# A fused attention and expert kernel on one core: first loads put first on their queue, the embeddings' small operations moved to the end of the attention, and the last two steps' products taken by row block

## The reference, cut to what matters

```python
scores = scale * np.matmul(q, k.transpose(0, 1, 3, 2))
thresh = np.max(scores, axis=-1, keepdims=True) - tau
scores = np.where(scores >= thresh, scores, -1000000000.0)
...
en = expert_emb / (np.linalg.norm(expert_emb, axis=-1, keepdims=True) + 1e-06)
logits = xn @ en.T / tau
...
g = h * np.tanh(sp)
return (g @ w_out).astype(np.float32)
```

## Time and profile before

| | |
|---|---|
| median of 3 executions | 1137.78 us (1134.08 to 1138.17) |
| the profiled execution, its time | 1136.53 us |
| the same execution, span from first to last instruction | 1134.9 us |
| PE busy | 1050.8 us, 93% |
| attention until about | 322 us |
| routing, then experts until about | 700 us |
| dense layer until | 1130 us |
| PE busy in 350 to 640 us | 262.67 of 290 us |
| PE busy in 640 to 1120 us | 460.50 of 480 us |

### The profile page before, as it was taken

How to read it: one execution, slowest core, us unless ns; L and a number is a source line. 1 busy time by engine, 2 the same in 40 slices (tenths; PEclk the granted TensorE clock), 3 DMA queues, 4 the chain that set the end, 5 groups by cost and what they waited for, 6 DMA issues and landing times.

```text
span 1134.9 us, 21943 instructions
## 1 busy us (share of the span) xinstructions
PE 1050.8 (93%) x6536; PEld 873.3 (77%) x6536; DVE 634.9 (56%) x1477; ACT 508.5 (45%) x1035; POOL 584.8 (52%) x680
## 2 busy tenths in 40 slices
PE   7999999999985997789999995799999999999998
PEld 5676777777753876668888884699999999999997
DVE  6888878787844511112222221567767667676664
ACT  4676667676654211112222221345554554545553
POOL 3322223232375777777762431886656556565554
PEclk9999999999996999899999998999999999999999
DMA  3452313231355898998882632520101001010000
GB/s 79 145 144 61 97 39 98 60 87 50 98 163 179 251 297 254 293 298 280 267 282 82 226 117 83 179 73 1 57 1 56 1 0 55 0 55 0 29 1 29
DMA packets 102621, 129.56 MB, mean 114 GB/s; under 512 B 39520, under 2 KB 56928, under 8 KB 102048
## 3 DMA queue, kind: packets, MB, share of 16 engines
q1 hardware_dynamic: 78912, 68.39, 20.3%
q0 software_dynamic: 18880, 53.22, 15.1%
q10 hardware_dynamic: 4768, 7.15, 1.7%
HBM read 112.74 MB, written 15.99 MB: 113 GB/s over the span
## 4 chain that ended last, share of the span: by engine, by line
PE 55%; POOL 7%; DMA 6%; issue 3%; DVE 2%; ACT 0%; POOLq 0%; DVEq 0%; SPq 0%; ACTq 0%
PE ps L1003 17%; PE ps L1002 17%; PE ps L1001 17%; DMA stage<-w 5%; POOL wl L525 3%; PE ps L1027 1%; POOL woutl L525 1%; POOL xs_far L556 1%; POOL wh L536 1%; PE ps L941 1%; POOL xs_near L556 1%; DMA wouth<-w_out 1%; PE ps L1077 1%; PE ps L997 1%; PE ps L951 0%
## 5 line engine op out<-in xcount | busy, mean ns | idle before, releaser
L525 POOL TENSOR_TENSOR wl<-stage,wh 128x512 fp32r<-128x512 f32 x128 | 161.3, 1291 | 57.0 <-DMA stage<-w 56.2
L637 POOL TENSOR_TENSOR mg<-mw,mr 128x384 f32<-128x384 f32 x96 | 118.4, 1233 | 74.9 <-DVE mr L1407 74.8
L682 ACT ACTIVATE ex<-sc,rmin 128x576 f32<-128x576 f32 x144 | 111.6, 776 | 93.2 <-DVE sc L1187 92.7
L1001 PE MATMUL ps<-yth,winh 128*128 128x384 f32 x384 | 132.5, 345 | 7.5 <-DVE mw L1395 7.5
L641 POOL TENSOR_TENSOR gl<-mg,gh 128x384 fp32r<-128x384 f32 x96 | 97.6, 1017 | 77.0 <-ACT gh L813 77.0
L496 POOL TENSOR_SCALAR thr<-rmin,taup 128x1 f32<-128x1 f32 x144 | 71.5, 497 | 123.2 <-DVE sc L1187 123.2
L1187 DVE TENSOR_SCALAR_CACHE_REDUCE sc<-ps,nscale 128x576 f32<-128x576 f32 x144 | 117.0, 814 | 28.4 <-PE ps L856 23.5
L1003 PE MATMUL ps<-yth,winl 128*128 128x384 f32 x384 | 130.7, 340 | 0.0
L1002 PE MATMUL ps<-ytl,winh 128*128 128x384 f32 x384 | 130.0, 339 | 0.0
L1002 PE MATMUL ps<-woutl,gh 128*128 128x512 f32 x288 | 114.5, 397 | 0.0
L1003 PE MATMUL ps<-wouth,gl 128*128 128x512 f32 x288 | 114.4, 397 | 0.0
(11 more groups left out here) (198 smaller groups left out, 2373.3 us busy)
## 6 DMA issues: line engine op xcount, KB each, us to landing
wh<-w POOLq DMA_DIRECT2D x32, 1024.0 KB, 8.7
stage<-w SPq DMA_DIRECT2D x128, 256.0 KB, 4.5
y_sorted<-yo ACTq DMA_DIRECT2D x25, 256.0 KB, 4.2
q_t<-qT SPq DMA_DIRECT2D x16, 288.0 KB, 2.9
k_t<-kT SPq DMA_DIRECT2D x16, 288.0 KB, 3.0
vb<-v SPq DMA_DIRECT2D x16, 288.0 KB, 3.4
out<-os SPq DMA_DIRECT2D x18, 256.0 KB, 2.8
stage<-w_in SPq DMA_DIRECT2D x16, 256.0 KB, 3.2
```

The lines of the kernel that those rows point to most:

```text
L525: g.tensor_tensor(dst, raw, src.bitcast(F32), ALU.subtract).then_inc(w_split, 1)
L637: g.tensor_tensor(mg[:, f % 2, :], mw[:, f % 2, :], mr[:, f % 2, :], ALU.mult).then_inc(g_done, 1)
L682: act.activation(ex[:, i % 2, t * S:(t + 1) * S], sc[:, i % 2, t * S:(t + 1) * S], ACT.Exp, bias=rmin[:, i % 2, t:t + 1], scale=-1.0).then ...
L1001: pe.matmul(out_, lhs_h, rhs_h, start=start, stop=False)
```

## The change

Four things are altered. On SP the loads of both taus and of the embeddings go to the head of ACT's list, and `q_d` gets a semaphore of its own, `qd_in`, for which only the fifth unit's scores wait. On PE `scores(0, 0)` comes ahead of the embeddings' products. On DVE only the copy of the norms (`ne`) stays at the beginning, behind `copy_max(0, 0)`; the rest goes in two pieces in front of the last two units' `norm`. And `down` of the last two steps of the last group is written out by row block, each finished block counting on `tail_done`, for which its `rows_out` waits.

```diff
     @block.sync
     def _(sp):
-        sp.dma_start(tauc[:, :], tau).then_inc(tau_in, 16)
-        sp.dma_start(mtau[:, :], moe_tau).then_inc(tau_in, 16)
-        sp.dma_start(emb[:, :, :], embT.rearrange("(k p) e -> p k e", p=P)).then_inc(emb_in, 16)
         def load(t, par):
             sp.dma_start(q_t[:, par, :], q_rows[t]).then_inc(qk_in[par], 16)
             sp.dma_start(k_t[:, par, :], k_rows[t]).then_inc(qk_in[par], 16)
-            sp.dma_start(q_d[0:DH, par, 0:DH], qT[t, 0, :, PAIRS * P:S]).then_inc(qk_in[par], 16)
-            sp.dma_start(q_d[DH:P, par, DH:P], qT[t, 1, :, 0:DH]).then_inc(qk_in[par], 16)
+            sp.dma_start(q_d[0:DH, par, 0:DH], qT[t, 0, :, PAIRS * P:S]).then_inc(qd_in[par], 16)
+            sp.dma_start(q_d[DH:P, par, DH:P], qT[t, 1, :, 0:DH]).then_inc(qd_in[par], 16)
...
     @block.scalar
     def _(act):
+        act.dma_start(tauc[:, :], tau).then_inc(tau_in, 16)
+        act.dma_start(emb[:, :, :], embT.rearrange("(k p) e -> p k e", p=P)).then_inc(emb_in, 16)
+        act.dma_start(mtau[:, :], moe_tau).then_inc(emb_in, 16)
...
+        exp(0, 0)
         act.wait_ge(norms_e, 2)
         act.activation(er0[:, :], ne[:, :], ACT.Ln).then_inc(ln_e, 1)
         act.wait_ge(ln_e, 1)
         act.activation(er1[:, :], er0[:, :], ACT.Exp, scale=0.5).then_inc(rec_e, 1)
-        exp(0, 0)
         exp(0, 1)
...
             if j == 0:
-                pe.wait_ge(qk_in[st], (body + i // BODY) * 64 + 64)
+                pe.wait_ge(qk_in[st], (body + i // BODY) * 32 + 32)
             wait(pe, max_done, tiles_before(body, i))
             if tiles_of(i) == 1:
+                pe.wait_ge(qd_in[st], (body + i // BODY) * 32 + 32)
...
+        scores(0, 0)
         pe.wait_ge(cvec, 2)
+        pe.wait_ge(const_gp, 5)
         for k in range(KD):
             m = pe.matmul(ps[:, INV0:INV0 + E], ones[:, :], embsq[:, k, :], start=k == 0, stop=k == KD - 1)
         m.then_inc(norms_e, 1)
-        scores(0, 0)
         scores(0, 1)
...
-        for f in range(NF - LAG, NF):
+        for f in range(NF - LAG, NF - 2):
             down(NG - 1, f, False)
+
+        def down_rows(f, j):
+            pe.wait_ge(gl_ready, (NG - 1) * NF + f + 1)
+            m = passes(ps[:, 2048 + 512 * j:2560 + 512 * j], gh[:, f % 4, j * P:(j + 1) * P],
+                       gl[:, f % 4, j * P:(j + 1) * P], wouth[:, f, :], woutl[:, f, :], False, f == NF - 1)
+            if f == NF - 1:
+                m.then_inc(tail_done, 1)
+
+        for f, j in ((NF - 2, 0), (NF - 2, 1), (NF - 1, 0), (NF - 1, 1), (NF - 2, 2), (NF - 1, 2)):
+            down_rows(f, j)
...
-        dve.wait_ge(tau_in, 32)
+        dve.wait_ge(tau_in, 16)
...
-        dve.wait_ge(emb_in, 16)
+        dve.wait_ge(emb_in, 32)
...
+                if last and i == BODY - 2:
+                    emb_recip()
+                if last and i == BODY - 1:
+                    emb_scale()
                 norm(b, i)
...
             copy_max(0, i, 1)
+            if i == 0:
+                emb_norms()
...
-        dve.wait_ge(down_done, NG * NF)
         for j in range(GT_):
+            dve.wait_ge(tail_done, j + 1)
             rows_out(NG - 1, j)
```

More of the change, by code:

```diff
@@ L245, in build @@
     qk_in = [sem(f"qk_in{i}") for i in range(2)]
+    qd_in = [sem(f"qd_in{i}") for i in range(2)]
     v_in = [sem(f"v_in{i}") for i in range(2)]
@@ L331, in build @@
     os_ready = sem("os_ready")
+    tail_done = sem("tail_done")
     out_stored = [sem(f"out_stored{j}") for j in range(GT_)]
@@ L1165, in norm_recip, with emb_norms, emb_recip, emb_scale @@
             link(dve.reciprocal(out_, r2))
[L1167 to L1179, removed]
+        def emb_norms():
+            dve.wait_ge(norms_e, 1)
+            dve.tensor_copy(ne[:, :], ps[:, INV0:INV0 + E]).then_inc(norms_e, 1)
+        def emb_recip():
+            dve.wait_ge(rec_e, 1)
+            norm_recip(ne[:, :], er0[:, :], er1[:, :], er2[:, :], er0[:, :])
+            link(dve.reciprocal(rtau[:, :], mtau[:, :]))
+        def emb_scale():
+            link(dve.tensor_scalar(er2[:, :], er0[:, :], rtau[:, :], None, ALU.mult))
+            dve.tensor_tensor(embn[:, :, :], emb[:, :, :], er2[:, :].unsqueeze(1).to_broadcast([P, KD, E]),
+                              ALU.mult).then_inc(emb_scaled, 1)
+            dve.wait_ge(const_gp, 7)
+            dve.tensor_scalar(tri_b[:, :], tri[:, :], -1.0, None, ALU.add)
+            dve.tensor_copy(ones_b[:, :], ones[:, :])
+            dve.tensor_copy(lane_b[:, :], lane_f[:, :])
         def copy_max(body, i, t):
```

## The result

The changed kernel is slower: 1140.3 us, the median of 22 executions (1136.75 to 1143.25), against 1137.12 us for the kernel before in 22 of its own, a ratio of 1.0032 with a 95% interval from 1.0021 to 1.0042. The profiled execution took 1142.28 us, its span 1140.6. The forecast was 1133.0, in a range from 1130.5 to 1136.0.

What follows compares the result with a forecast made beforehand. PE, busy 93% of the span, was taken as the bound. 2.74 us at the beginning plus 1.05 at the tail made 3.8 off the profiled 1136.53, or 1132.7, put at 1133.0 us for the median; range 1130.5 to 1136.0.

Steps and rivals of the forecast that it cites:

- The end of the attention: Last two units' norms: moved VectorE operations, 1.5 and 1.1 us, hidden in 2.37 and 1.68 us of idleness.
- the moved operations are not hidden: Rival at the attention's end: both moved pieces cost their full length, 2.6 us, giving 1135.5 us; chance 0.05.
- Slower than before: Rival: without early small products PE stays slow beyond the third unit; four units, 9 us, give 1142; chance 0.05.
- The beginning: Program start: first scores 2.94 us earlier through earlier loads, 2.74 us after the reordering's cost.
- keys' landing: Program start: first keys land 3.2 us after issue, at 4.65 us; bounds 2.8 to 3.6 us.
- The reordering: Program start: small products after the first scores delay the second unit's scores by 0.20 us.
- TensorE's pace: First units' scores: pace changes at the same unit, costing nothing; at most 1.05 us lost if the third is slow.
- The new wait: Each fifth unit's scores: the `qd_in` wait costs nothing; otherwise 0.8 us over 16 steps.
- The tail: Program end: one copy after the last product, 1.21 us less, against a 0.16 us stall; worth 1.05 us.
- The sum: Whole kernel: 2.74 us at the beginning plus 1.05 at the tail, 3.8 us gained; put at 1133.0 us.

Runs made afterwards that it cites:

- e3: The kernel before with only VectorE's small operations moved to the attention's last two units; ratio 1.0066 to the kernel before.
- e5: The changed kernel with VectorE's moved operations placed in the attention's first body instead of its last; ratio 0.9981 to the kernel before.
- e1: The changed kernel with GpSimd's first low parts held back until VectorE has done the moved operations; ratio 1.0005 to the kernel before.
- e4: The kernel before with four extra, unused GpSimd subtractions of 128x512 added near the start; ratio 1.0023 to the kernel before.
- e8: As e5, but ScalarE issues the three small loads only when the first queries and keys are in; one execution, no ratio, first scores at 4.60 us.
- e2: The kernel before with only the new tail, the last two steps' products by row block; ratio 0.9993 to the kernel before.
- e7: The changed kernel with only the three conversions in the first body, the chain of nine operations left at the attention's end; ratio 1.0027 to the kernel before.
- e6: As e5, with the first step's keys issued at the head of ScalarE's list; ratio 0.9979 to the kernel before, median 1132.97 us.

## Why the prediction was wrong

**The step that failed** is the one headed "The end of the attention". It took the moved operations' durations from the beginning, 1.5 and 1.1 us, and laid them into 2.37 and 1.68 us of VectorE's idleness. The idleness was there. The durations were not: beside GpSimd's subtractions the two groups take 4.7 and 5.4 us, so that the last norm comes 5.95 us later after the eighth than before (10.65 - 4.70), where no delay was forecast. e3 adds this and nothing else and gets 5.55 us later at `inv_i`; e5 takes it out and gets 5.3 back; e1 and e4 show that GpSimd's work, not the place, sets the durations. The prediction never asked what GpSimd does at that time. The rival "the moved operations are not hidden" had the right place and capped the price at 2.6 us, since it too took the old durations. "Slower than before" was given 0.05, on a slow pace of TensorE at the beginning that did not occur; that its 1142 us lies near the measured 1140.3 is coincidence.

The Trainium skill bears on this and could have warned of it ("SBUF — State Buffer", section "Who interferes with whom"). It says that VectorE and GpSimd share one pair of SBUF ports, that an operation of GpSimd holds it for the whole instruction, and which VectorE operations need it: copies, casts and `tensor_scalar` out of SBUF in the modes that use both ports, and operations with two SBUF inputs against a GpSimd operation that reads SBUF; reductions do not. The traces agree at each of these points: 0.17 to 1.19 us for `tensor_scalar` and `tensor_tensor`, 0.22 to 1.3 for casts, `TENSOR_REDUCE` 0.30 in both cases, copies out of PSUM 0.17. The traces add that eight columns are enough, and that reciprocals, which the section does not name, are not held up (0.20). The trace of before may be read as the same thing turned round, which no run was made to test: GpSimd's threshold on one column takes 0.3 us, and 0.87 when VectorE's mask starts beside it; here from the changed kernel's POOL timeline, in which the mask of 13.18 to 14.00 us lies beside the second row and VectorE reads PSUM beside the first.

```profile
12.54 0.28 POOL L495 TENSOR_SCALAR thr<-rmin,taup 128x1 f32<-128x1 f32 x1 [1.17 <-DVE sc L1208]
13.28 0.87 POOL L495 TENSOR_SCALAR thr<-rmin,taup 128x1 f32<-128x1 f32 x1 [0.46 <-DVE sc L1208]
```

**The beginning** was right in mechanism and too large: by a fifth at its own places, by more further on. Forecast were 2.94 us for the first scores and 2.74 after the reordering; measured 2.43 and 2.34 at those places, and 1.7 at `inv_i` in e5. The mis-sized term is the keys' landing: 3.2 us forecast, 3.8 to 4.2 measured with the small loads on ScalarE's queue, 3.2 without them (e8). It lay outside the bound of 3.6 at the upper end. The prediction took it that the small packets had delayed the keys before, from SP's queue; the keys' 3.2 us were the same behind them on one queue (before) and without them (e8), so nothing of that shows. The starting point was also high: other executions of the old beginning have the first scores at 7.19, 7.08 and 6.42 instead of 7.59.

**The reordering** cost 0.1 us at the second unit's copy, 0.2 forecast. TensorE's pace rose within the third unit's scores: they took 1.47 us, against 2.29 in the first two and 1.24 from then on. Before, that unit's scores, at 15.47, already took 1.24, so 0.2 us of the 1.05 held in reserve for this was spent on TensorE; the five records of the transposes before it were slow too (1.27 us against 0.74). VectorE didn't feel it: its third unit's copy starts at 15.02 instead of 17.34, still 2.32 us early.

**The new wait** `qd_in` cost nothing: from the first scores to the last norm it is 315.1 us in e5 with it, and 314.9 and 315.4 with the old waits in the kernel before and in e2.

**The tail**: 1.05 us forecast. In the rows 1.34 less after the last product, against a stall of (1136.77 - 1132.64) - (1129.73 - 1125.88) = 0.28 over the last 18 products, where 0.16 was forecast: 1.06.

**The sum.** By the rows the changed kernel should be 3.59 - 1.06 = 2.5 us slower; the medians say 3.2, the ratio's interval 2.4 to 4.8. **Open:** e7 is at `inv_i` 1.9 us late and has the new tail, which makes 0.9 us or 1.0008; its measured interval begins at 1.0011. e1, e3 and the changed kernel also lie 1.1 to 1.9 us above what `inv_i` and tail make. The other five lie 0 to 1.0 us above it, and each interval is 2.4 to 4 us wide. From `inv_i` to the last product single executions differ by several us (777.0 in e6, 781.8 in e5), so the traces don't tell. One thing goes with it: the mean granted clock of all timed executions is 0.9715, 0.9729, 0.9712 and 0.9724 in the changed kernel, e1, e3 and e7, the four with operations left at the attention's end, and 0.9742 to 0.9752 in the others and in the kernel before. In the changed kernel, e3 and e7 a part of that is the stretch at 0.50 from about 321 us on, which lies before `inv_i` and so is counted already. Whether the rest costs what is missing, and why e1 has it, no run shows.

## What to carry to other kernels

Idle time on an engine is not room for an operation: ask what the neighbours do in that time, and take the operation's duration from a row with the same neighbours. Here a short VectorE operation that read two SBUF operands, or converted or scaled out of SBUF, lasted until the GpSimd subtraction beside it had ended, 1.2 to 1.3 us for work of 0.2; put such work where GpSimd rests, or read from PSUM. Where a difference of a few us is lost in the scatter of whole executions, two or three milestones in the timeline tell the parts from one another, and a kernel with one part alone settles what a sum only suggests.

## What the runs showed of the hardware that was not expected

- An operation of VectorE on 128 x 8 float32 took 0.15 to 0.17 us alone and up to 1.19 beside GpSimd's subtractions of 128 x 512 (1.23 us each); reciprocals of the same size 0.20 in both cases. Each slow operation ended about 0.1 us or less after one of the subtractions.
- After 2.76 us without work TensorE ran the attention's last products at its lower level: in the changed kernel, e3 and e7 the granted clock reads 0.50 then, and twenty records took 1.27 to 1.34 us, against 0.80 in the other kernels, where it had been idle for 0.47 to 0.53 us.
- Holding GpSimd back by 4.4 us brought a collision of the same kind some 18 us further down the program, for 2.2 us (e1).
- Three small loads issued from a second queue at the same time delayed two loads of 288 KB by 0.56 to 0.95 us, and took 3.4, 3.9 and 3.9 us themselves, where ahead of them on one queue they took 2.0, 2.0 and 2.2. The Trainium skill ("DMA: Bandwidth & Descriptors", section "Issuing engines are not separate DMA queues") says that transfers of different engines interleave on the same DMA engines; e6 and e8 agree.
